# A linear-attention and two-MLP kernel on one core: another order of the work before the first slot, and another preparation of each tile

## The reference

```python
mag = np.sqrt(a_re * a_re + a_im * a_im)
scale = np.minimum(mag, 0.999) / (mag + 1e-06)
a_re_n, a_im_n = (a_re * scale, a_im * scale)
for t in range(S):                                   # S = 768, per batch (4) and head (8), D = 48
    S_re, S_im = ar * S_re - ai * S_im, ar * S_im + ai * S_re
    S_re += k_t v_t^T;  y_t = q_t^T S_re
h = x @ w_in                                         # 3072 tokens x 384 -> 2048
x = (np.maximum(h, 0.0) + np.log1p(np.exp(-np.abs(h)))) @ w_out
out = ((x @ w1) * (x @ w2) @ w3) @ w_out2            # 384 -> 1024 -> 384
```

## Time and profile before

| | us |
|---|---|
| median of 3 runs | 982.48 (980.43 to 983.35) |
| the profiled execution | 982.79 |
| its span | 981.0 |
| TensorE busy | 920.0 (94%) |
| VectorE busy | 599.0 (61%) |
| ScalarE busy | 436.1 (44%) |
| mean granted TensorE clock | 0.974 of 2.4 GHz |

### The profile page before, as it was taken

One profiled execution on the slowest core, in us unless ns is written; L12 is line 12 of the kernel. 1 busy time (PEld: TensorE's weight loads), 2 busy tenths in 40 slices (PEclk: granted clock), 3 DMA queues, 4 the chain that ended last, 5 costly groups with the idle time before them and its releaser, 6 DMA issues.

```text
span 981.0 us, 14349 instructions
## 1 busy us (share of the span) xinstructions
PE 920.0 (94%) x5352; PEld 811.1 (83%) x5352; DVE 599.0 (61%) x976; ACT 436.1 (44%) x619; POOL 70.5 (7%) x58
## 2 busy tenths in 40 slices
PE   4995939999999999999999999999999999999998
PEld 1554839989989989989899999999788888888887
DVE  4968678989898998898999832355221212121211
ACT  5262254585674674664764654587102020202011
POOL 0000000000000000000000000000222222222221
PEclk9997669999999999999999999999999999999999
DMA  9477066273372391480570550421101010101000
GB/s 336 181 213 237 20 194 134 78 195 91 109 173 83 109 220 38 141 210 14 157 195 13 143 114 14 147 90 46 36 1 65 1 64 1 64 0 64 0 33 33
DMA packets 97878, 99.50 MB, mean 101 GB/s; under 512 B 6928, under 2 KB 88848, under 8 KB 97808
## 3 DMA queue, kind: packets, MB, share of 16 engines
q1 hardware_dynamic: 97808, 98.59, 34.8%
HBM read 63.96 MB, written 29.88 MB: 96 GB/s over the span
## 4 chain that ended last, share of the span: by engine, by line
PE 67%; DVE 17%; ACT 5%; DVEq 4%; DMA 3%; issue 3%; SPq 1%; ACTq 1%
PE ps_p L1345 7%; PE ps L1345 7%; PE ps L1347 7%; PE ps L1346 7%; PE ps_p L1347 7%; PE ps_p L1346 7%; PE ps_ay L1407 4%; DVE sp L1223 2%; PE ps_ay L1347 2%; PE ps_ay L1346 2%; PE ps_ay L1345 2%; DMA w3s<-in_w3t 2%; PE ps_k L1347 2%; PE ps_k L1345 2%; PE ps_k L1346 2%
## 5 line engine op out<-in xcount | busy, mean ns | idle before, releaser
L1345 PE MATMUL ps<-g_h,wo_h 128*128 128x384 f32 x384 | 132.8, 346 | 2.2 <-DVE g_l L1230 2.2
L666 POOL TENSOR_TENSOR abl<-ab,abh 128x512 fp32r<-128x512 f32 x48 | 69.1, 1440 | 903.4 <-DVE abh L1328 903.4
L1347 PE MATMUL ps<-g_h,wo_l 128*128 128x384 f32 x384 | 129.1, 336 | 0.0
L1346 PE MATMUL ps<-g_l,wo_h 128*128 128x384 f32 x384 | 128.8, 335 | 0.0
L1345 PE MATMUL ps_p<-x1h,win_h 128*128 128x384 f32 x336 | 116.8, 348 | 6.0 <-DVE sp L1223 6.0
L1347 PE MATMUL ps_p<-x1h,win_l 128*128 128x384 f32 x336 | 112.6, 335 | 0.0
L1346 PE MATMUL ps_p<-x1l,win_h 128*128 128x384 f32 x336 | 112.5, 335 | 0.0
L1319 DVE TENSOR_TENSOR ab<-ps_ay,bc 128x512 f32<-128x512 f32 x24 | 16.6, 692 | 114.1 <-ACT bc L953 114.1
L775 ACT ACTIVATE sp<-ps_p 128x768 f32<-128x768 f32 (+1 forms) x63 | 46.2, 733 | 86.2 <-PE ps_p L1347 86.2
L788 ACT ACTIVATE g_h<-sp 128x768 fp32r<-128x768 f32 (+1 forms) x71 | 55.3, 779 | 65.0 <-DVE sp L1223 64.6
L1319 DVE TENSOR_TENSOR ab<-ps_p,bc 128x512 f32<-128x512 f32 x24 | 16.6, 692 | 103.1 <-ACT bc L953 103.1
(11 more groups left out here) (167 smaller groups left out, 2037.0 us busy)
## 6 DMA issues: line engine op xcount, KB each, us to landing
qk_scr<-tt SPq DMA_DIRECT2D x16, 576.0 KB, 5.4
stq<-qk_scr SPq DMA_DIRECT2D x48, 192.0 KB, 4.8
qk_scr<-pp SPq DMA_DIRECT2D x16, 576.0 KB, 4.2
stk<-qk_scr SPq DMA_DIRECT2D x48, 192.0 KB, 4.6
an<-in_a_re SPq DMA_DIRECT2D x8, 576.0 KB, 4.1
an<-in_a_im SPq DMA_DIRECT2D x8, 576.0 KB, 5.5
qk<-in_q SPq DMA_DIRECT2D x8, 576.0 KB, 7.7
qk<-in_k SPq DMA_DIRECT2D x8, 576.0 KB, 9.3
```

Of the source, the lines that this page charges most:

```text
L666: tensor_tensor(abl[:, m % AR, :], ab[:, m % 2, :], abh[:, m % AR, :].bitcast(F32), ALU.subtract).then_inc(ab_lo, 1)
L1345: mm(o, wh, xh, start=start, stop=False)
L1346: mm(o, wh, xl, start=False, stop=False)
L1347: return mm(o, wl, xh, start=False, stop=stop)
```

## The change

It has two parts.

In the prologue: the first mask comes after run 5 of tile 1 and no longer after run 7, a weight piece's low part, the ends and the first carry, which go between the later pieces of the attention; the low parts of pieces 6 and 7 are made there too, and their high parts on ScalarE a piece of the attention earlier or later; the keys of tile 0 end after tile 1's m2; ScalarE makes tile 0's inverse before `raw_low_out(2)`; SyncE loads a of tile 1 before weight piece 5; tile 1's queries are multiplied behind x1's low part.

In every preparation: the carries work on pairs of runs ("carry in" multiplies the ends within pairs, steps 1 to 16 go over the 24 pairs, "carry out" gives the other half: seven products of half the width for six). "Scale start" is gone; for tiles 2 to 7 its operation is `prep_root_less` on ScalarE, and so are the three copies of the ends (`prep_ends`). The inverse is split around the mask of step 5. The beginning of tile n+3's preparation moves later: squares behind the last output copy, m2 behind x1's low part, log, root and square around the high part of step 7, Newton behind step 7's low part, and scale and the first "a" between the sum and the low part of the next tile's step 0.

```diff
-            for i in range(3, 6):
+            for i in range(3, 5):
                 load_piece(i)
             wait(prep_p, 2)
             load_a(1)
             store_q(0, first=True)
+            load_piece(5)
...
+            def prep_ends(m):
+                carries = gp[:, :, :].rearrange("p c (g r) -> p c g r", g=G)
+                ends = an[:, :, :].rearrange("p c (g k i r) -> p c g k i r", g=G, i=RUN, r=CR)
+                most = (NCH - 1) * CR
+                eng.wait_ge(runs_made, m + 1 - IN_SLOTS)
+                for c in range(2):
+                    act(carries[:, c, :, 1:1 + most].rearrange("p g (k r) -> p g k r", r=CR),
+                        ends[:, c, :, 0:NCH - 1, RUN - 1, :], ACT.Copy)
+                act(carries[:, :, :, 1 + most:NR], ends[:, :, :, NCH - 1, RUN - 1, 0:CR - 1], ACT.Copy).then_inc(ends_out, 1)
+
+            def prep_root_less(m):
+                eng.wait_ge(prep_root_made, m + 1 - IN_SLOTS)
+                act(te[:, 0, :], te[:, 1, :], ACT.Copy, bias=-1e6).then_inc(prep_less, 1)
...
             w34_rows(4)
+            prep_inverse(0)
             raw_low_out(2)
-            prep_inverse(0)
             w34_rows(5)
...
-            for i in range(4, 7):
+            for i in range(4, 6):
                 raw_high(i)
-                if i <= BY_PE:
-                    raw_low_out(i - 1)
+                raw_low_out(i - 1)
+            raw_low_out(5)
             k_by_tokens(0, 0)
             for i in range(NG):
                 if i + 1 < NG:
                     k_by_tokens(0, i + 1)
                 y_out(0, i, first=True)
-                if i == 1:
-                    raw_high(7)
-            prep_psquares(1)
+                if i in (0, 2):
+                    raw_high(6 + i // 2)
 
             eng.wait_ge(raw_lo, 8)
-            for part in range(2):
-                y_loaded(0, part)
-                x1_high(0, part, first=True)
+            y_loaded(0, 0)
+            x1_high(0, 0, first=True)
+            prep_psquare(1, 0)
+            y_loaded(0, 1)
+            x1_high(0, 1, first=True)
+            prep_psquare(1, 1)
...
             g_high(0, 0, False)
+            prep_root_less(2)
...
                     if has_prep and j == 5:
                         prep_inverse(n + 2)
+                    if has_prep and j == 2:
+                        prep_ends(n + 2)
...
-                        if nxt_prep and j == 5:
-                            prep_squares(n + 3)
                         g_high(n, j + 1, split)
                     elif j == NP1 - 2:
                         if nxt_prep:
-                            prep_log(n + 3)
-                            prep_root(n + 3)
+                            prep_squares(n + 3)
                         if nxt:
                             for part in range(2):
                                 y_loaded(n + 1, part)
                                 x1_high(n + 1, part)
+                        softplus(n, j + 1, split)
                         if nxt_prep:
-                            prep_root_square(n + 3)
-                        softplus(n, j + 1, split)
+                            prep_log(n + 3)
                         g_high(n, j + 1, split)
+                        if nxt_prep:
+                            prep_rsqrt(n + 3)
                     elif nxt:
                         softplus(n + 1, 0, False)
+                        if nxt_prep:
+                            prep_root_less(n + 3)
                         g_high(n + 1, 0, False)
...
             def prep_scale(m):
-                ve.scalar_tensor_tensor(out=tr[:, :], in0=te[:, 1, :], scalar=-1e6, in1=tr[:, :],
-                                        op0=ALU.add, op1=ALU.mult)
+                if m < IN_SLOTS:
+                    ve.tensor_scalar(te[:, 0, :], te[:, 1, :], -1e6, None, ALU.add)
+                    eng.drain()
+                else:
+                    eng.wait_ge(prep_less, m + 1 - IN_SLOTS)
+                ve.scalar_tensor_tensor(out=tr[:, :], in0=te[:, 1, :], scalar=1.0 / 0.999, in1=te[:, 0, :],
+                                        op0=ALU.min, op1=ALU.mult)
...
+            def prep_carry_in():
+                t = gp[:, :, :].rearrange("p c (a l) -> p c a l", l=2)
+                n = GC * CR // 2
+                m1 = ms[:, 0:2 * n].rearrange("p (c a) -> p c a", c=2)
+                m2 = ms[:, 2 * n:4 * n].rearrange("p (c a) -> p c a", c=2)
...
-                w = NR - s_
+                w = NPAIR - s_
                 m1 = ms[:, 0:2 * G * w].rearrange("p (c g r) -> p c g r", c=2, g=G)
-                m2 = ms[:, 2 * G * NR:2 * G * NR + 2 * G * w].rearrange("p (c g r) -> p c g r", c=2, g=G)
-                cmul(carries[:, 0, :, s_:], carries[:, 1, :, s_:], carries[:, :, :, s_:],
-                     carries[:, 0:1, :, 0:w].to_broadcast([P, 2, G, w]), carries[:, 1:2, :, 0:w].to_broadcast([P, 2, G, w]),
+                m2 = ms[:, 2 * G * w:4 * G * w].rearrange("p (c g r) -> p c g r", c=2, g=G)
+                cmul(pairs[:, 0, :, s_:], pairs[:, 1, :, s_:], pairs[:, :, :, s_:],
+                     pairs[:, 0:1, :, 0:w].to_broadcast([P, 2, G, w]), pairs[:, 1:2, :, 0:w].to_broadcast([P, 2, G, w]),
...
+            def prep_carry_out():
+                v = gp[:, :, :].rearrange("p c (g m l) -> p c g m l", g=G, l=2)[:, :, :, 1:, 0]
+                w = NPAIR - 1
+                m1 = ms[:, 0:2 * G * w].rearrange("p (c g r) -> p c g r", c=2, g=G)
+                m2 = ms[:, 2 * G * w:4 * G * w].rearrange("p (c g r) -> p c g r", c=2, g=G)
+                done = pairs[:, :, :, 0:w]
+                cmul(v[:, 0], v[:, 1], v, done[:, 0:1].to_broadcast([P, 2, G, w]), done[:, 1:2].to_broadcast([P, 2, G, w]), m1, m2)
...
-            before_mask = {0: steps("a", 1), 1: steps("run", 3, 4), 2: steps("run", 7) + ["ends"] + steps("carry", 1),
-                           3: steps("carry", 8, 16, 32), 4: by[3:] + ["p"], 5: []}
-            after_mask = {0: steps("run", 1), 1: steps("run", 5), 2: steps("carry", 2), 3: by[:2], 4: [("q", 0)], 5: ["inverse"]}
-            after_sum = {0: steps("run", 2), 1: steps("run", 6), 2: steps("carry", 4), 3: by[2:3], 4: [("q", 1), "p2"], 5: ["keys"]}
+            before_mask = {0: steps("a", 1), 1: steps("run", 3, 4), 2: steps("run", 7) + ["ends", "carry in"],
+                           3: steps("carry", 8, 16) + ["carry out"], 4: by[3:] + ["p"], 5: ["inverse start"]}
+            after_mask = {0: steps("run", 1), 1: steps("run", 5), 2: steps("carry", 1), 3: by[:2], 4: [("q", 0)], 5: ["inverse end"]}
+            after_sum = {0: steps("run", 2), 1: steps("run", 6), 2: steps("carry", 2, 4), 3: by[2:3], 4: [("q", 1), "p2"], 5: ["keys"]}
...
+            prep(0, True, ["m2", "newton", "scale"] + steps("a", 0, 1) + steps("run", 1, 2, 3, 4, 5, 6, 7) +
+                 ["ends", "carry in"] + steps("carry", 1, 2) + steps("carry", 4, 8) + steps("carry", 16) + ["carry out"] + by +
+                 ["p", ("q", 0), ("q", 1), "p2", "inverse start", "inverse end", "keys"], first=True)
+            prep(1, False, ["m2"])
+            prep(0, True, ["keys end"])
+            prep(1, False, ["newton", "scale"] + steps("a", 0, 1) + steps("run", 1, 2, 3, 4, 5))
             mask_scores(0, 0)
-            between = [steps("carry", 2), steps("carry", 4), steps("carry", 8), steps("carry", 16), steps("carry", 32),
-                       by[:1], by[1:2], by[2:3], by[3:], [], ["p"], []]
+            between = [steps("run", 6), steps("run", 7), ["ends", "carry in"], steps("carry", 1, 2), [], steps("carry", 4, 8),
+                       steps("carry", 16) + ["carry out"], [], by[:1], by[1:2], by[2:3], by[3:] + ["p"]]
             for i in range(NG):
                 if i + 1 < NG:
                     mask_scores(0, i + 1)
                 prep(1, False, between[2 * i])
                 new_state(0, i, ps_z0)
                 prep(1, False, between[2 * i + 1])
-                if i == 2:
-                    raw_low(7)
-            prep(1, False, steps("q", 0, 1))
+                if i in (1, 3):
+                    raw_low(6 + i // 2)
             x1_low(0)
-            prep(1, False, ["p2", "inverse", "keys", "keys end"])
+            prep(1, False, ["p2", ("q", 0), ("q", 1), "inverse start", "inverse end", "keys", "keys end"])
             prep(2, True, ["m2"])
...
+            prep(2, True, ["newton"])
             g_low(0, 0, False)
+            prep(2, True, ["scale"] + steps("a", 0))
...
                     if nxt_prep and j == 6:
-                        prep(n + 3, not even, ["newton"])
+                        prep(n + 3, not even, ["m2"])
                     if j < NP1 - 1:
                         add_relu(n, j + 1, split)
                     elif nxt:
+                        add_relu(n + 1, 0, False)
                         if nxt_prep:
                             prep(n + 3, not even, ["scale"])
-                        add_relu(n + 1, 0, False)
                     if has_prep and j < 6:
```

(6 more changed lines are left out.)

72 lines of the change are left out of this document (42 added, 30 removed).

## The result

The changed kernel takes 992.85 us in the median of 16 runs (984.34 to 996.40), the kernel before 983.29 on the same chip (16 runs, 979.87 to 986.57). The ratio is 1.0093, with a 95% interval of 1.0073 to 1.0114: slower by 0.9%, 9 us. Forecast were 976 and faster. The profiled execution took 996.4 (span 994.6, mean clock 0.962), 13.6 more than that of before.

What follows compares the result with a forecast made beforehand. TensorE and VectorE were taken as nearly full in the slots, with TensorE's other idle time before 150 us. Prologue -13.4, slots +4.0, clock +2.6 give -6.8 against 982.79: 976 us, 972 to 980 for this case alone, range 965 to 985.

Steps and rivals of the forecast that it cites:

- The prologue's order: Prologue: first mask 8 us sooner, TensorE resumes for tile 1's scores at 134.7 instead of 148.06; -13.4 us.
- the 113.3 of the sum: Tile 0's attention: VectorE's queue ends last, so x1's low part is ready at 113.3 us, 13.6 us sooner.
- Three waits go and one new stop of 2.9 us forms: Slot boundaries: waits of 0.49, 0.65, 0.59 go, TensorE stops 2.9 for step 0's low part; +2.5 us in five slots.
- The sum's 290.1: Slot boundary: TensorE, without its waits, arrives at 290.1 us for step 0's low part, which is ready at 293.0.
- 1.5 for the split inverse: Odd-tile slots: "inverse start" ahead of step 5's mask makes the sum 0.35 to 0.7 later; +1.5 us in three slots.
- Two falls in five, 1.3 us each: Slot boundaries: the new stop brings the clock down at two of five; +2.6 us, bounds 0 and 9.9.
- The slower one: Rival: clock falls once in tile 0's attention and at the beginning of slots 1 to 5; +3.7, 986 us; chance 0.12.
- the prediction's zero for it: Slots: copies of the ends cost nothing, scale start's removal is covered, shorter carries save VectorE 1.1 us a preparation.

Runs made afterwards that it cites:

- kernel 1: The changed kernel with only the work at the boundary between two slots put back as before; 974.59 us, ratio 0.9920 to the kernel before.
- kernel 3: The kernel before with only the change's prologue order; boundary, inverse, ends and six-step carries as before; 974.68 us, ratio 0.9924 to the kernel before.
- kernel 9: The changed kernel with both boundary stops filled by unread matmuls, 4 ahead of the scores and 9 ahead of down(n+1,0); 983.93 us, ratio 1.0018.
- kernel 13: The changed kernel with only the 2.2 us stop ahead of down(n+1,0) filled, by 9 unread matmuls; 982.06 us, ratio 1.0006 to the kernel before.
- kernel 2: The changed kernel with only the prologue's order put back as before; 999.49 us, ratio 1.0162 to the kernel before.
- kernel 14: The changed kernel with only the 1.1 us stop ahead of the scores filled, by 4 unread matmuls; 986.90 us, ratio 1.0051 to the kernel before.
- kernel 8: The changed kernel with ScalarE's boundary order and VectorE's m2 put back as before, the rest of VectorE's boundary order as changed; 989.94 us, ratio 1.0067.
- kernel 11: The changed kernel with the boundary as before, three prologue stops filled with 12, 22 and 54 unread matmuls, inverse whole; 973.29 us (972.92 with it split).
- kernel 12: The changed kernel with the boundary order put back, but scale's subtraction kept on ScalarE behind step 7's high part; 977.77 us, ratio 0.9953.
- kernel 4: The changed kernel with step 0's low part ahead of scale and a, and its high part ahead of ScalarE's subtraction; 986.28 us, ratio 1.0047.
- kernel 5: The changed kernel with both boundary stops filled by too many unread matmuls, 7 ahead of the scores and 14 ahead of down(n+1,0); 988.38 us, ratio 1.0059.

## Why the prediction was wrong

**The prologue's order: right, with the other clock.** First mask at 83.5: TensorE waited 0.79 for it, as said. x1's low part was there at 117.5 for the 113.3 of the sum, and tile 1's scores at 138.7 for 134.7. The prediction had named the condition: 138 if the clock falls after 97. It fell in the us from 97 to 98, behind a stop of 2.88 where 2.6 were expected. I had put that at 4 in 10. So -9.3 in the trace stands for -13.4. In the traces of kernels 1 and 3 the clock fell there too but came back within the attention, and the scores started at 136.2 and 135.8; in time the new prologue is worth 7.5 to 8 us.

**"Three waits go and one new stop of 2.9 us forms": right in kind, short in size.** The three waits went (but for x1's in slot 4). The new stop came in two parts, 1.1 and 2.2, 3.3 together. The chain from the last up product to step 0's low part took 17.4 us for the 16.5 that I had summed. The difference is one link that the sum left out, the transfer of y, for which ScalarE waits before x1's second high part:

```profile
272.70 0.85 ACT L768 ACTIVATE x1h<-x1raw 128x768 fp32r<-128x768 f32 x1 [0.61 <-PE ps_p L1407]
274.41 0.53 ACT L768 ACTIVATE x1h<-x1raw 128x384 fp32r<-128x384 f32 x1 [0.86 <-DMA x1raw<-ys]
```

Before, log and root stood ahead of these two and the transfer was hidden. Moved away, they uncovered it: both high parts went through in one row, without such a wait, in the earlier trace rows. The sum's 290.1 for TensorE's arrival is also 0.25 us short of its own terms (276.47 and 13.88). I had priced these edits at +4.0, 2.5 of it for this stop, 0.5 a slot, and 1.5 for the split inverse. Kernels 9 and 13, which have the stops and not the falls, say 8 to 10, 1.5 to 2.0 a slot; the missing link is 0.9 of the difference, and for the rest no step is shown.

**"Two falls in five, 1.3 us each": the step that failed, together with the price of the stop.** The two terms priced the boundary at 6.6 us, and it took 17. The clock fell at all five boundaries in the trace, and the falls cost 7 to 9 us, not 2.6. This term alone doesn't turn the sign: with the falls at 8 and all else as forecast the sum is -1.4, with the stops at 9 and all else as forecast -1.8. With both, and the prologue at 7.8 for 13.4, it is +9. Both factors of the clock's term were off. The frequency: I compared the stop with the two isolated ones of the earlier trace rows, after 2.5 and 3.4 us of idling. Here two stops lie close together with only the scores between them, and this pair brought the fall at all ten boundaries of two traces (the changed kernel and kernel 2), where 2.2 us alone did so at two of five boundaries in kernel 14 and at four in kernel 8. The size: I took half of 3.95 us, and less in odd slots. The stretch at half clock is 6.8 us long, 5 to 6 of it work. Nor does a slot with an odd tile hide more of it: from trace to trace the four measured slots grew by 3.5, 4.2, 4.0 and 4.3 us in turn.

**The rivals.** The slower one had the mechanism: a fall in tile 0's attention and one at each of slots 1 to 5, 986. It got 0.12. What it lacked to 993 is the stops' other 4 to 6 us. The Trainium skill ("TensorE: Matmul & The Clock Gate", section "HAM oscillation — how this bites in real kernels") tells of a fall in every round of a loop whose waits between bursts are 3 to 5 us long. I had stretched that to a stop of 2.9 us, which it doesn't say. The two stops measured here, 1.1 and 2.2 us, are shorter still, and the clock fell five times in five: the pattern is the page's, the lengths are not.

**The part "shorter preparation".** Its work did get shorter and was worth nothing, as the prediction's zero for it says; the split inverse cost the predicted 0.6 us in slots with an odd tile, but taking it back changed neither the slot nor the time (kernel 11).

What stays open: why a stop of 2.2 us alone brings the clock down at one boundary and not at another; what makes up the rest of the stops' price, 8 to 10 us where 2.5 was forecast; where the other half of kernel 11's 0.6 us goes; and in how far kernel 12's loss is the late copies or its later soft-plus.

## What to carry to other kernels

An in-order engine has idle gaps ahead of the work that the bound engine waits for. Here work was taken out of such a gap and put "later, where it is needed"; it landed between two such pieces of work, and the bound engine paid for it; look at which gap a step fills before moving it. Sum the chain with every link, the transfers that the moved work used to hide among them. And price TensorE's new stops with the clock: a pair of short ones cost here about as much again in clock as in waiting, 7 to 9 us beside 8 to 10.

## What the runs showed of the hardware that I had not expected

- A stop of 1.1 us and one of 2.2 with the scores (1.5 us) between them brought the clock to 0.50 for 6.8 us at five boundaries of five; 2.2 alone for 3.4 us at two of five (kernel 14) and at four of five (kernel 8); 0.5 to 1.1 alone at none of five (kernel 13). With kernel 4's pair of 0.4 to 0.9 and 1.4 it fell at four of five, once only some 6 us later. Each count is of one execution.
- Plain fp32 matmuls of 96x128 by 128 columns kept the clock at 1.00 through these stops (kernels 5, 9 and 13). A record of theirs is 0.118 us after the last, one of the scores' 0.14 (eight in 1.13).
- 54 such matmuls in a 13 us stop made the 6.5 us after it full speed, 2.4 to 2.7 us in the trace; the times show 1.7, within their intervals.
- Executions of the same kernel differ by what TensorE spends at half clock: mean clock 0.962 to 0.979 and 996 to 984 us in the changed kernel.
